# A fused attention and two-layer network kernel: from one head at a time to pairs of heads with block-diagonal queries

## What is computed

```python
scores = scale * q @ k^T + min(-(cum[i] - cum[j]), 0)      # cum = cumsum(max(s, 0)), causal mask
attn   = exp(scores - max) / (sum + 1e-9)                  # B=4, H=8, S=576, D=64, all fp32
x      = (attn @ v), heads laid side by side               # [2304, 512]
h = x @ w_in;  x = (h * cos(h)) @ w_out                    # 512 -> 2048 -> 512       (stage B)
xn = x / rms(x) * g                                        #                          (stage C)
out = (silu(xn @ w_gate) * (xn @ w_val)) @ w_out2          # 512 -> 1536 -> 512
```

## Time and profile before

| | |
|---|---|
| runs | 1214.45, 1217.87, 1220.16 us; median 1217.87 |
| profiled execution | span 1214.9 us; its device time is not listed apart from the three runs |
| PE busy | 1186.0 us, 98% of the span |
| DVE, ACT, POOL busy | 745.1, 622.2, 354.8 us |
| attention | from the start to 322.85 us, the end of the last product with v |

### The profile page before, as it was taken

The page is one execution under the profiler, slowest core; times in us unless marked ns, Lnnn a source line. Parts: engine busy times, 40 slices in busy tenths (PEclk is TensorE's granted clock), DMA queues, the critical chain, the costliest instruction groups (busy, mean ns, idle before and its releaser), DMA issues.

```text
span 1214.9 us, 25276 instructions
## 1 busy us (share of the span) xinstructions
PE 1186.0 (98%) x8511; PEld 1098.9 (90%) x8511; DVE 745.1 (61%) x1826; ACT 622.2 (51%) x1554; POOL 354.8 (29%) x473
## 2 busy tenths in 40 slices
PE   6999999999999999999999997999999999999998
PEld 4888888888899999999999897999999999999997
DVE  7989898988785555655556687534344444443432
ACT  4788777877656555655556463223323322332221
POOL 6788888877760000000000399200000000000000
PEclk9999999999999999999999999999999999999999
DMA  5333343332230000000000044000000000000000
GB/s 125 86 91 95 87 102 93 82 97 62 72 102 1 1 2 1 0 0 0 0 0 0 28 122 123 17 19 1 17 17 0 17 0 17 17 0 17 0 18 18
DMA packets 91393, 46.94 MB, mean 39 GB/s; under 512 B 60816, under 2 KB 81296, under 8 KB 91344
## 3 DMA queue, kind: packets, MB, share of 16 engines
q1 hardware_dynamic: 91344, 46.31, 13.9%
HBM read 41.49 MB, written 4.79 MB: 38 GB/s over the span
## 4 chain that ended last, share of the span: by engine, by line
PE 89%; DVE 6%; ACT 2%; issue 2%; POOL 0%; DMA 0%; SPq 0%; DVEq 0%; POOLq 0%; ACTq 0%
PE psum L1259 26%; PE psum L1215 14%; PE psum L1166 14%; PE psum L1271 12%; PE psum L1152 7%; PE psum L1131 6%; PE psum L1102 6%; PE psum L1085 4%; DVE b_r L808 2%; DVE b_lo L819 1%; PE psum L1107 1%; DVE b_r L805 1%; ACT b_c L548 1%; ACT b_r L545 1%; DVE b_g L814 0%
## 5 line engine op out<-in xcount | busy, mean ns | idle before, releaser
L1259 PEld LDWEIGHTS psum<-c_x,cw 128*128 128x128 f32 x2592 | 322.8, 191 | 7.1
L1259 PE MATMUL psum<-c_x,cw 128*128 128x256 f32 x2592 | 326.5, 283 | 0.0
L1215 PE MATMUL psum<-b_hi,wout 128*128 128x288 f32 x1024 | 227.1, 297 | 11.7 <-DVE b_lo L819 11.7
L1215 PEld LDWEIGHTS psum<-b_hi,wout 128*128 128x128 f32 x1024 | 171.9, 189 | 14.2 <-DVE b_lo L819 13.7
L905 DVE TENSOR_TENSOR c_t<-psum,c_t 128x256 f32<-128x256 f32 x108 | 45.9, 425 | 191.7 <-ACT c_t L651 191.7
L1215 PE MATMUL psum<-b_lo,wout 128*128 128x288 f32 x512 | 151.2, 295 | 0.0
L651 ACT ACTIVATE c_t<-psum 128x256 f32<-128x256 f32 x108 | 41.5, 384 | 207.7 <-PE psum L1259 207.6
L1271 PE MATMUL psum<-cw,c_hi 128*128 128x512 f32 x432 | 135.2, 394 | 0.0
L1042 POOL TENSOR_SCALAR cw<-stage 128x512 fp32r<-128x512 f32 x36 | 26.8, 745 | 333.5 <-PE psum L1166 323.4
L1152 PE MATMUL psum<-pT_hi,vs 128*128 128x320 f32 (+3 forms) x448 | 113.5, 312 | 0.0
L1166 PE MATMUL psum<-bx_odd,win 128*128 128x288 f32 x768 | 112.8, 295 | 0.2 <-ACT c_rms L572 0.2
(11 more groups left out here) (108 smaller groups left out, 2054.6 us busy)
## 6 DMA issues: line engine op xcount, KB each, us to landing
cum_row<-cum_rows SPq DMA_DIRECT2D x32, 288.0 KB, 3.4
stage<-in_moe_w_out SPq DMA_DIRECT2D x28, 256.0 KB, 2.6
out<-stage SPq DMA_DIRECT2D x18, 256.0 KB, 2.1
raw_q<-in_q SPq DMA_DIRECT2D x32, 128.0 KB, 2.2
raw_k<-in_k SPq DMA_DIRECT2D x32, 128.0 KB, 2.3
raw_v<-in_v SPq DMA_DIRECT2D x32, 128.0 KB, 2.3
stage<-in_moe_w_in SPq DMA_DIRECT2D x16, 256.0 KB, 2.6
stage<-in_moe_w_gate SPq DMA_DIRECT2D x12, 256.0 KB, 2.8
```

The lines of the kernel that those rows point to most:

```text
L1215: last = mm(Y_BANKS[f][:, 0:TB], wout[j][:, a, cols], g[j % 4][:], start=(j == 0 and m == 0), stop=(j == NJ - 1 and m == 2))
L1259: last = mm(GV_BANKS[c % 3][:, n * TC:(n + 1) * TC], weights(c, a)[:, kc], c_x[:, b, kc], start=(kc == 0 and m == 0), stop=(kc == KC - 1 a ...
```

## The change

The host now lays q and k out turned over, and the weights in the order in which they are used. Attention goes over 16 pairs of heads, with nine query tiles of 64 rows. The stationary operand of a score product holds the queries of two heads block-diagonally (head 0 in rows and columns 0 to 63, head 1 in 64 to 127), so one product with the stacked keys of both heads gives both heads' scores, in three passes. The front's transposes, `make_bias` and the copies for them are gone: the key's cumulated sum alone is added (`cum8`), since a row's constant drops out of the softmax. The probabilities are not normalised; x is multiplied by 1/sum at the end (POOL `normalise`), with the row of inverses turned by a round trip through DRAM (SP `turn_inverse`). v has two half-zero copies for each pair (`vv`), so that both heads add into one PSUM region of 576 columns in three passes. There is one `prob` buffer, two score banks, and one x region. Each engine goes through one pass for each p: the nine tiles of pair p, with the second half of the transposes and the product with v of pair p - 1 between them. Three `up` of stage B's tile 0 run inside the last attention pass, and 24 weight pieces (10 of `w_in`, 14 of `w_out`) are split in that tile, high parts by ACT (`tile_piece`), low parts by POOL.

```diff
-QT_N = 5
-TILE_ORDER = [4, 3, 2, 1, 0]
-QROWS = [128, 128, 128, 128, 64]
+NP = NH // 2
+QT = SEQ // HD
+TILE = [QT - 1 - n for n in range(QT)]
+KEYS = [HD * (i + 1) for i in range(QT)]
...
+            for p in range(NP + 1):
+                now, before = p < NP, p >= 1
+                if now:
+                    logits(p, 0)
+                if before:
+                    evac_lo(p - 1, 2)
+                    sum_plus_eps(p - 1)
+                if now:
+                    logits(p, 1)
+                if before:
+                    row_inverse(p - 1)
+                    evac_lo(p - 1, 3)
...
+            def split_qk(p):
+
+                b = p % 2
+                at_least(pool, qk_loaded[b], 16 * ((p + 1) // 2))
+                if p >= 2:
+                    at_least(pool, scores_done, QT * (p - 1))
+                nc.gpsimd.tensor_scalar(qk[b][:, 0, :], raw[b][:, 0:QK_COLS], 1.0, 0.0,
+                                        ALU.mult, ALU.add).then_inc(qk_hi, 1)
+                at_least(pool, qk_hi, p)
+                nc.gpsimd.tensor_tensor(qk[b][:, 1, :], raw[b][:, 0:QK_COLS], qk[b][:, 0, :].bitcast(F32),
+                                        ALU.subtract).then_inc(qk_lo, 1)
...
+            def scores(p, n):
+
+                i = TILE[n]
+                if p == 0 and n in (0, 2):
+                    pe.wait_ge(first_lo, 1 if n == 0 else 2)
+                elif n == 0:
+                    at_least(pe, qk_lo, p)
+                at_least(pe, logits_ready, QT * p + (n - 1 if n >= 2 else n))
+                src = qk[p % 2]
+                at = SEQ + n * P
+                spans = score_spans(n)
+                for b, lo, hi in spans:
+                    diag = hi >= KEYS[i]
+                    for m, (a, k) in enumerate(((0, 0), (0, 1), (1, 0))):
+                        mm(psum[:, b, 0:hi - lo], src[:, a, at:at + P], src[:, k, lo:hi],
+                           start=(m == 0), stop=(m == 2 and not diag))
...
+            def times_v(p, a):
+
+                at_least(pe, pT_lo_ready, 4 * p + 4)
+                at_least(pe, v_lo, p + 1)
+                if a == 0:
+                    at_least(pe, x_stored, p)
...
+                part(0, -1, 3, O_AT - HD, True, True)
+                part(0, 2, 7, y_at, True, False)
+                part(1, 2, 7, y_at, False, False)
+                part(2, 4, 5, y_at + 2 * HD, False, False)
+                part(3, 6, 3, y_at + 4 * HD, False, False)
+                last = part(4, 6, 3, y_at + 4 * HD, False, True)
...
+            for p in range(NP + 1):
+                now, before = p < NP, p >= 1
+                if now:
+                    scores(p, 0)
+                if before:
+                    prob_T(p - 1, 2)
+                if now:
+                    scores(p, 1)
+                else:
+                    pe.wait_ge(bx_lo, 1)
+                    pe.wait_ge(logits_ready, QT * NP)
+                    up(0, 0, 0)
+                if before:
+                    prob_T(p - 1, 3)
+                if now:
+                    scores(p, 2)
+                    scores(p, 3)
+                else:
+                    up(1, 1, 0)
+                if before:
+                    times_v(p - 1, 0)
+                if now:
+                    scores(p, 4)
+                    prob_T(p, 0)
+                    scores(p, 5)
+                else:
+                    up(2, 2, 0)
+                if before:
+                    times_v(p - 1, 1)
+                if now:
+                    scores(p, 6)
+                    prob_T(p, 1)
+                    scores(p, 7)
+                    scores(p, 8)
```

More of the change, by code:

```diff
@@ L90, in sem @@
             return ctx.enter_context(nc.semaphore(name))
+        EARLY = 4
+        pieces = [("in", j) for j in range(EARLY)]
+        for j in range(NJ):
+            pieces.append(("out1", j))
+            if j + EARLY < NJ:
+                pieces.append(("in", j + EARLY))
+        N_B = len(pieces)
+        for c in range(NC2):
+            pieces += [("gate", c), ("val", c), ("out2", c)]
+        NPIECES = len(pieces)
+        NUMBER = {piece: n for n, piece in enumerate(pieces)}
         xT = sb("xT", [P, KC, TOKENS], F32)
@@ L282, in per_head @@
[L282 to L302 removed]
+        BX_HI_STEP, BX_LO_STEP = 8, 10
+        IN_ATTENTION = EARLY + 2
@@ L419, in _ @@
-            run_steps(sp, step)
-            sp.wait_ge(in_lo, NJ)
-            for n in range(NPIECES):
+            for p in range(NP):
+                if 1 <= p and p + 1 < NP:
+                    load_cum(p + 1)
+                if p >= 1:
+                    turn_inverse(p - 1)
+                if p + 3 < NP:
+                    load_qk(p + 3)
+                    load_v(p + 3)
+                if 1 <= p <= IN_ATTENTION:
+                    load_piece(p - 1)
+            for n in range(IN_ATTENTION, IN_ATTENTION + 3):
+                load_piece(n)
@@ L422, in _ @@
+            turn_inverse(NP - 1)
+            for n in range(IN_ATTENTION + 3, NPIECES):
                 load_piece(n)
@@ L762, in evac_lo @@
+            def evac_lo(p, u):
+                at_least(dve, pT_hi_ready, 4 * p + u + 1)
+                for (src, dst), (_, hi) in zip(unit_moves(u, pT_lo), unit_moves(u, pT_hi)):
+                    last = nc.vector.tensor_tensor(dst, src, hi.bitcast(F32), ALU.subtract)
                 last.then_inc(pT_lo_ready, 1)
@@ L1138, in _ @@
-            PV = [[(1, 0, 320, 2, 1088), (1, 128, 320, 3, 1408), (1, 128, 320, 4, 1600)],
-                  [(1, 0, 320, 1, 768)],
-                  [(0, 0, 256, 0, 0), (0, 64, 256, 1, 576), (1, 0, 320, 0, 256)]]
-            def times_v(h, par, part):
-                at_least(pe, pT_lo_ready, 4 * h + 2 + part)
-                if part == 0:
-                    at_least(pe, v_lo, h + 1)
-                for n, (b, lo, hi, kb, at) in enumerate(PV[part]):
-                    rows = 64 if kb == 4 else P
-                    first = par == 0 and part != 1 and n == 0
-                    final = par == 1 and part == 2 and n > 0
-                    for m, (pv, pp) in enumerate(((0, pT_hi), (0, pT_lo), (1, pT_hi))):
-                        last = mm(O_BANKS[b][:, lo:hi], vs[par][0:rows, pv, kb, :], pp[0:rows, at:at + hi - lo],
-                                  start=(first and m == 0), stop=(final and m == 2))
-                last.then_inc(pv_done, 1)
```

922 lines of the change are left out of this document (414 added, 508 removed).

## The result

The changed kernel takes 1281.27 us as the median of four runs (1279.37 to 1282.82), the kernel before 1217.77 (four runs beside them): a ratio of 1.0525, 95% interval 1.0505 to 1.0545. The change costs 63.5 us (66.0 between the profiled spans), 16 more than the 47.5 of my sum, and the time lies in the range.

A forecast was written before the change was run, and what follows sets the result against it. The prediction took one chain through ACT, DVE and PE, no longer PE, to bound attention. Attention's end +46, passage to stage B -0.5 and tile 0 +2 make +47.5 us, 1265 on the median 1217.9; it took 1264, range 1222 to 1288.

The forecast's parts named there:

- round trip: Attention's chain of waits through ACT, DVE and PE, once around per pair: 19.9 us, of which PE works 13.3.
- A: From the end of a product with v through ACT's and DVE's evacuations, exponential and logits of tiles 7 and 8: 5.0 us.
- C: sum_plus_eps, logits, exponential, then high and low part of unit 3, ahead of times_v: 3.5 us.
- D: PE's part: times_v(p, 0), scores 4, five transposes, scores 5, times_v(p, 1): 6.8 us and 0.1 for the end.
- POOL: In attention, DVE's sum_plus_eps waits out POOL's long instruction: 23 us in all, bounds 0 and 60.
- The clock: PE's clock at 0.50 in parts of most attention passes, hitting scores(p+1,0) only: 14 us, range 0 to 56.
- Tile 0: Stage B's first tile, where ACT's six instructions a step come to 3.2 to 3.3 us: +2 us, between 0 and 8.
- 1: Rival: the chain, the waits on POOL and part of the clock, as summed: 1250 to 1282 us; chance 0.45.
- 2: Rival: the chain and the waits on POOL without clock loss: 1251 us; chance 0.12.
- 3: Rival: no waits on POOL, clock loss as taken: 1241 us; without either 1228; chance 0.20 together.
- 4: Rival: clock stays at 0.50 through both times_v of most passes: 1290 to 1320 us; chance 0.09.
- 5: Rival: shorter round trip, 1129 us at PE's own 13.3 a pair; chance 0.08 faster, 0.06 within 0.5%.

The follow-up runs named there:

- e6: e5 with ACT making the high part of unit 1 ahead of the exponential of tile 6: 1241.92 us.
- e10: e6 with e2's split, unread PE products, and scores(p,4) and prob_T(p,0) ahead of times_v(p-1,0), DVE's logits of tile 2 ahead of evac_lo(p-1,3): 1206.39 us.
- e2: The changed kernel with POOL's low part of q and k in four instructions of 432 columns in place of one of 1728: 1257.32 us.
- e5: The changed kernel with DVE's sum_plus_eps and row_inverse moved behind evac_lo(p-1,3): 1257.17 us.
- e11: e10 with two weight loads issued between the last inverses' store and load, and POOL's last normalise after four more low parts of pieces: 1202.81 us.
- e1: The changed kernel with sum_plus_eps adding a tile of constants by TENSOR_TENSOR in place of TENSOR_SCALAR with a constant: 1277.35 us.
- e12: e6 with e2's split, no unread PE products, and POOL's low part of a weight piece in tile 0 in four instructions of 128 columns: 1247.20 us.

## Why the prediction was right, point by point

- **PE no longer the bound; one round trip is.** Right. A took 5.1 us for 5.0, C 3.4 for 3.35. The full-clock pass without POOL, with A shortened by 1.0, is 19.06 to 19.13, so the round trip as it stood is 20.1 where I had 19.9. Shortening A by 1.0 (e6) took 0.8 off the mean pass, and D by 1.07 (e10) 1.06 off each. The 14 passes of the changed kernel, 322.5 us, can be added up from their parts (us):

| part of a pass | shortest | 14 passes above that |
|---|---|---|
| `scores(p, 0)` start to first logits | 1.20 | 5.3 |
| to `times_v(p - 1, 0)` | 6.72 | 16.3, equal to the waits for POOL |
| to `times_v(p - 1, 1)` | 4.22 | 18.5 |
| to its end | 2.88 | 0.1 |
| to the next `scores(p, 0)` | 5.15 | 0.0 |
| sum | 20.17 | 40.1 |

  The 5.3 and the 18.5 are there only in passes where the clock was at 0.50 in that part.
- **POOL.** The mechanism was right, and the size of the wait nearly: 18.9 us less 16 times 0.16, 16.3, for 23. In the passes behind a weight piece `sum_plus_eps` took 1.2 to 2.0 us, where I had a wait of 2.5. In pass 9, where I had 1.7 for the split of x, it took 2.4, and in pass 13, a plain one, 2.2: ahead of their splits of q and k, POOL stood 2.0 and 2.9 us for the inverses' DMA, which I had put down as covered. What I missed is that the wait is no sum of its own. Removing it gave 24 us (e2, e5), since PE's standing costs through the clock too.
- **The clock: the term that was mis-sized.** Predicted 14 us, on `scores(p+1, 0)` alone. Over 14 passes it measured 23.8 us. On these scores it is 5.3: up to 0.8 us a pass, near the 0.9 that I took, but not in every pass. The other 18.5 are in the part with `times_v(p, 0)` (4.1 us for 2.75 in the pass shown), which I had left out of the sum. What falls between the two is covered by ACT and DVE. The Trainium skill (TensorE: Matmul & The Clock Gate, "Why this matters for your kernels") warns only of gaps longer than those of this pass. The trace does not agree: the longest gap of the pass shown is 2.56 us, and the clock fell in every pass. The measurement decides.
- **Start.** First logits at 12.78 for 11.8; the first pass took 15.39 for 12.0. I had ACT's exponentials set its pace. PE went at the pace of 1.2 GHz at first: three products of 512 columns take 1.45 us (13.56 to 15.01), as they do from 143.92 inside a stretch at 0.53 (1.43), and the logits of the first tiles came 1.0 to 2.6 us apart behind them. The granted clock reads 1.00 for this time, so that it was the clock is read from the pace alone.
- **Passage to stage B.** -3.1 for -0.5. I kept the chain behind the last product as it was. Before, ACT waited 0.93 us there for the first `up`, done already now, and DVE's two all-SBUF instructions took 0.85 and 1.52 us beside POOL, where now they take 0.46 and 0.45: POOL is idle then, waiting for the inverses.
- **Tile 0.** +6.2 us (58.1 for 52.0) for +2, inside the 0 to 8. I named ACT's own work. The trace names the supply; chain of waits of the changed kernel, in order of time:

```profile
373.07 9.91 DMA inv_rows<-row_inv
383.00 0.49 SPq L392
...
383.53 4.01 DMA inv_row<-inv_rows
387.61 1.42 POOL xT L970
389.03 4.17 POOL w L978 x3
393.22 3.59 DMA stage<-in_w_in
```

  The store of 4-byte elements takes 9.9 us to land, with SP's weight loads queued behind it and POOL idle for 12.2. "Some 10 us of slack" covers it in most passes (POOL waited for the inverses in six, 6.2 us in all) and not behind the last one. e11 took 3.2 us off e10's 59.4, and the 56.2 left are 4.2 above the kernel before; I did not take them apart. Nor did I follow why the same tile took 57.1 to 62.3 us in e1 to e10.
- **The last tile** took 61.5 us for 58.8, unforeseen. It took 58.6 to 60.5 in the experiments, with the same instructions; the changed kernel has two stretches of 6.8 us at 0.50 there, the kernel before one of 3.4. What decides that is open.
- **Rivals.** 1 is what happened, at the upper end. 2 (no clock loss) is excluded by e12, 3 (no waits for POOL) by the 1561 ns and e5. 4 (0.50 through both `times_v`) did not happen: from `times_v(p, 1)` to its end it is 2.88 us in every pass. 5 (a shorter round trip, down to PE's own work) is excluded by the 20.17, and PE was busy for 103.24 of 140.1 us, 49.9 to 190.
- **What was luck.** The total came within the range by errors that partly cancel. Against the sum, the 14 passes were longer by 11 us through the clock and 4 through the round trip, the start and first pass by 4.4, tile 0 by 4 and the last tile by 2.7; the waits for POOL were 7 us shorter and the passage 2.6.

Stretch of the changed kernel, columns as above:

```profile
49.90:190.00 140.10, 103.24 (x603) 91.32 (x602) 56.26 (x151) 55.44 (x144) 66.21 (x54) 0.85 0.30 86
```

## What to carry to other kernels

Fewer products gain little once no engine works ahead: with single buffers, follow the one round trip through all engines before counting any engine's work. Here the half that was missing was order, not work: three changes of order, POOL's instruction in four, a few products to hold the clock and two weight loads sooner took the same arithmetic from 1281 to 1203 us. A short DVE instruction with all its data in SBUF can cost what POOL's longest instruction lasts, so put it where nothing waits behind it, and price a stand of PE twice, once as time and once through the clock of the work that follows.

## What the runs showed of the hardware that I had not expected

- DVE's TENSOR_TENSOR on nine SBUF columns waits POOL out as TENSOR_SCALAR does (1500 and 1561 ns on average); the reads from PSUM do not (957 ns for 768 columns, in each run).
- PE stood for no longer than 2.56 us in the pass shown, and was at 1.2 GHz for a quarter of attention (27 stretches, 99 of some 370 us); where the stretch falls decides its price: 1.6 us on the product with v, 0.8 on `scores(p, 0)`, nothing measurable on what ACT and DVE cover.
- In tile 0, beside DVE, POOL's two-input instruction takes 525 ns for 128 columns and 1356 for 512: three more instructions a piece cost 744 ns, some 250 each.
- A store of 1152 elements of 4 bytes took 9.9 us to land, where 256 KB in long rows took 2.6.
